# Splitting the output weights on TensorE while a delta-rule kernel inverts its first systems

## The reference, cut to what matters

```python
# attention by the delta rule, 2 x 8 heads, 768 tokens, head size 48
k_n = k / (np.linalg.norm(k, axis=-1, keepdims=True) + 1e-06)
for t in range(S):
    y[t] = q[t] @ state
    state = state + beta[t] * outer(k_n[t], v[t] - k_n[t] @ state)
# SoLU layer, 1536 rows, 384 -> 1024 -> 384
h = x @ w_in;  solu = h * softmax(h)
ln = (solu - mean) / sqrt(var + 1e-6) * g_ln
x = ln @ w_out
# router (x @ w_gate, best of 8) and one expert per row, 384 -> 1024 -> 384
```

## Time and profile before

| | us |
|---|---|
| median of 3 runs | 436.16 |
| lowest, highest | 435.88, 438.93 |
| the profiled execution, its own time | 435.01 |
| span of its records | 433.2 |
| PE busy, share of the span | 390.2, 90% |
| DVE busy | 311.4, 72% |
| ACT busy | 221.9, 51% |
| POOL busy | 66.6, 15% |

### The profile page before, as it was taken

The page is one execution under the profiler, slowest core; times in us unless marked ns, Lnnn a source line. Parts: engine busy times, 40 slices in busy tenths (PEclk is TensorE's granted clock), DMA queues, the critical chain, the costliest instruction groups (busy, mean ns, idle before and its releaser), DMA issues.

```text
span 433.2 us, 13384 instructions
## 1 busy us (share of the span) xinstructions
PE 390.2 (90%) x5617; PEld 371.1 (86%) x5618; DVE 311.4 (72%) x612; ACT 221.9 (51%) x393; POOL 66.6 (15%) x79
## 2 busy tenths in 40 slices
PE   3386789799999899999989998999999999999992
PEld 3386788779999888999877998999999999999991
DVE  6999699679957958883425887796596775647650
ACT  2437331647831226663124772577696594648650
POOL 3100200000020000010012000625144242210211
PEclk9999999999999969999999998999999999999997
DMA  7996001289100329101034941246738738080000
GB/s 152 328 227 176 5 2 36 50 160 314 70 34 10 74 70 209 34 21 40 5 77 123 395 175 38 56 145 225 285 76 305 249 129 315 26 309 21 25 5 26
DMA packets 27878, 54.37 MB, mean 125 GB/s; under 512 B 4468, under 2 KB 21424, under 8 KB 27344
## 3 DMA queue, kind: packets, MB, share of 16 engines
q1 hardware_dynamic: 23648, 48.04, 36.9%
q0 software_dynamic: 3136, 4.73, 3.5%
q10 hardware_dynamic: 1040, 0.79, 0.8%
HBM read 44.30 MB, written 9.44 MB: 124 GB/s over the span
## 4 chain that ended last, share of the span: by engine, by line
PE 74%; DVE 14%; issue 5%; SPq 2%; DMA 2%; ACT 1%; POOL 1%; POOLq 0%; DVEq 0%
PE PS L542 10%; PE PS L544 10%; PE PS L543 10%; PE PS L1509 8%; PE PS L1554 4%; PE PS L1564 3%; PE PS L1555 3%; PE PS L1438 3%; PE PS L1395 3%; PE PS L1424 2%; PE PS L1412 2%; PE PS L1521 2%; PE PS L1372 2%; SPq L269 2%; PE PS L1346 2%
## 5 line engine op out<-in xcount | busy, mean ns | idle before, releaser
L542 PE MATMUL PS<-xTh,w1h 128*128 128x224 f32 (+3 forms) x198 | 55.8, 282 | 0.6 <-DVE hTl L451 0.6
L543 PE MATMUL PS<-xTl,w1h 128*128 128x224 f32 (+3 forms) x198 | 55.5, 281 | 0.0
L544 PE MATMUL PS<-xTh,w1l 128*128 128x224 f32 (+3 forms) x198 | 55.5, 281 | 0.0
L1509 PE MATMUL PS<-w_in_h,mlpT 128*128 128x512 f32 x144 | 47.7, 404 | 0.9 <-DMA mlpT<-yT 0.7
L542 PE MATMUL PS<-w2h,hTh 128*128 128x384 f32 x136 | 46.2, 340 | 0.0
L544 PE MATMUL PS<-w2h,hTl 128*128 128x384 f32 x136 | 45.6, 335 | 0.0
L543 PE MATMUL PS<-w2l,hTh 128*128 128x384 f32 x136 | 45.5, 335 | 0.0
L451 DVE SCALAR_TENSOR_TENSOR hTl<-PS,hTh 128x384 fp32r<-128x384 f32 x64 | 35.5, 554 | 4.7 <-ACT hTh L349 4.7
L542 PEld LDWEIGHTS PS<-xTh,w1h 128*128 128x128 f32 x198 | 38.0, 192 | 1.0 <-DVE hTl L451 1.0
L477 POOL DMA_INDIRECT out<-yo,oiu x24 | 24.0, 999 | 92.6 <-ACT yo L360 84.7
L544 PEld LDWEIGHTS PS<-xTh,w1l 128*128 128x128 f32 x198 | 38.0, 192 | 0.0
(11 more groups left out here) (190 smaller groups left out, 908.6 us busy)
## 6 DMA issues: line engine op xcount, KB each, us to landing
w1r<-w SPq DMA_DIRECT2D x8, 1536.0 KB, 6.5
w2r<-w SPq DMA_DIRECT2D x8, 1536.0 KB, 10.8
KP<-kv SPq DMA_DIRECT2D x3, 1536.0 KB, 13.3
mlpT<-yT SPq DMA_DIRECT2D x12, 288.0 KB, 4.3
QT<-qt SPq DMA_DIRECT2D x6, 384.0 KB, 6.4
out<-zero SPq DMA_DIRECT2D x12, 192.0 KB, 3.9
x<-rowst SPq DMA_DIRECT2D x12, 192.0 KB, 1.9
XE<-w_out_t SPq DMA_DIRECT2D x1, 1536.0 KB, 6.4
```

The costliest lines, as they stand in the source:

```text
L542: pe.matmul(out_ap, lhs[0], rhs[0], start=first, stop=False)
L543: pe.matmul(out_ap, lhs[0], rhs[1], start=False, stop=False)
L544: return pe.matmul(out_ap, lhs[1], rhs[0], start=False, stop=final)
L1509: last = pe.matmul(PS[:, h_bank(n) + s, :], mlpT[:, n, x, c, :], w[:, c, o], start=(c == 0 and j == 0), stop=(c == KD - 1 and j == 2))
```

## The change

1. PE makes the low part of `w_out`: for each of 8 slices it multiplies the identity with the scaled `w_out` (f32, 384 columns) and the negated identity (`minus`) with `w_out_h` (fp32r), both into one PSUM bank, in four calls `w_out_low(0..3)` of two slices. ACT copies each call's result to `w_out_l`. ACT makes `w_out_h` in two halves. The subtraction at L1207 shrinks to the 64 columns of the router's part.
2. New orders. PE: `w_out_low(0)`, `w_out_low(1)`, `fold`, `w_out_low(2)`, `grams(1)`, `w_out_low(3)`, a wait for ACT's last copy, 8 products of zeros, `between(0)`, 4 products of zeros, `lower_block(0)`. `grams(1)` waits for ACT's part of `fold`. ACT: `w_out_high(0)`, `w_out_high(1)`, the copies of `w_out_low(0)` and `(1)`, `fold`, copy 2, `w_in_high` (moved up from `attention(0)`), copy 3, `odd_blocks(1)`, `between(0, 0)`, `lower_rows(0)`, `between(0, 1)`, `lower_block(0)`, `cross_blocks(1)`, `roots(1)`. DVE: after `place_rows(0)` a copy of block 1 that was ACT's, `scale_v(0)`, a wait for ACT's `lower_rows(0)`, a memset of block 3 that was POOL's, `lower_block(0)`, and only then `systems(1)` and `mask_first`.
3. The joining products go in halves of 16 units, so that the taking out of one half lies beside the products of the other; this holds for all groups.
4. The norms: ACT computes the square with the epsilon and the plain sum in two small instructions after the root (`Square` and `Identity` with a bias tile `tiny`), in place of two of DVE's.
5. `T1u` is stored as [block position, unit] in place of [unit, block position]: DVE's transposition writes in order, and PE reads its 32 columns 128 bytes apart.
6. The first DVE memset of PSUM is cut in halves, so that `grams(0)` waits for the first only; the copies of its odd blocks are cut in quarters, the first two taken half-way through the products.
7. SP issues `g_ln` and `w_out` first, then the keys of group 1, `w_gate`, `w_out_t`, `kv`, `w_in`.

```diff
+                sp.dma_start(gl[:], g_ln).then_inc(ld_wo, 16)
+                sp.dma_start(w_raw[:, :, 0:DM], w_out.rearrange("(k p) n -> p k n", p=P)).then_inc(ld_wo, 16)
+                load_kt(1)
+                sp.dma_start(wg[:], w_gate.rearrange("(c p) e -> p c e", p=P)).then_inc(ld_wt, 16)
                 sp.dma_start(w_out_t_sb, w_out_t.rearrange("(c p) f -> p c f", p=P)).then_inc(ld_wt, 16)
-                sp.dma_start(wg[:], w_gate.rearrange("(c p) e -> p c e", p=P)).then_inc(ld_wt, 16)
-                sp.dma_start(gl[:], g_ln).then_inc(ld_wt, 16)
-                sp.dma_start(w_raw[:, :, 0:DM], w_out.rearrange("(k p) n -> p k n", p=P)).then_inc(ld_wt, 16)
-                load_kt(1)
                 load_kv(0)
...
-                act.activation(nq[:], flat[:, 0:BL * BL:BL + 1], ACT.Sqrt).then_inc(root_done, 1)
+                act.activation(nq[:], flat[:, 0:BL * BL:BL + 1], ACT.Sqrt).then_inc(root_step, 1)
...
+                act.activation(nq2[:], nq[:], ACT.Square, bias=tiny[:]).then_inc(root_done, 1)
+                act.activation(nq1[:], nq[:], ACT.Identity, bias=tiny[:]).then_inc(root_done, 1)
...
 (ACT's list)
+                act.wait_ge(ld_wo, 32)
+                w_out_high(0)
+                w_out_high(1)
+                w_out_low(0)
+                w_out_low(1)
                 fold()
+                w_out_low(2)
+                w_in_high()
+                w_out_low(3)
                 odd_blocks(1)
+                between(0, 0)
                 lower_rows(0)
-                between(0)
+                between(0, 1)
+                lower_block(0)
+                cross_blocks(1)
                 roots(1)
-                cross_blocks(1)
-                lower_block(0)
...
 (DVE's list)
                 place_rows(0)
+                dve.wait_ge(td_ready, 1)
+                dve.tensor_copy(TT64[block(1), :, 1], TT64[block(1), :, 0]).then_inc(d_tb, 1)
                 scale_v(0)
+                dve.wait_ge(e_tb, 1)
+                dve.memset(TT64[block(3), :, 0], 0.0).then_inc(z_tt, 1)
+                lower_block(0)
+                systems(1)
                 mask_first()
-                systems(1)
-                lower_block(0)
                 dve.wait_ge(w_hi, 1)
-                dve.tensor_tensor(w_out_l[:], w_raw, w_out_h[:].bitcast(F32), ALU.subtract).then_inc(w_lo, 1)
+                dve.tensor_tensor(w_out_l[:, :, DM:RW], w_raw[:, :, DM:RW], w_out_h[:, :, DM:RW].bitcast(F32), ALU.subtract).then_inc(w_lo, 1)
...
 (PE)
+                def w_out_low(i):
+
+                    pe.wait_ge(w_main, i // 2 + 1)
+                    if i >= 2:
+                        pe.wait_ge(w_low_main, i - 1)
+                    for k in range(2 * i, 2 * i + 2):
+                        at = low_at(i)[:, k % 2]
+                        pe.matmul(at, ident[:], w_raw[:, k, 0:DM], start=True, stop=False)
+                        last = pe.matmul(at, minus, w_out_h[:, k, 0:DM], start=False, stop=True)
+                    last.then_inc(w_diff, 1)
...
+                w_out_low(0)
+                w_out_low(1)
                 fold()
+                w_out_low(2)
                 grams(1)
+                w_out_low(3)
+                pe.wait_ge(zero_ready, 1)
+                pe.wait_ge(w_low_main, 4)
+                idle_products(8)
                 between(0)
+                idle_products(4)
                 lower_block(0)
```

More of the change, by code:

```diff
@@ L720, in clear_t @@
                 def clear_t(g):
[L722 to L725, removed]
+                    if g == 0:
+                        pool.wait_ge(d_tb, 1)
+                    for c in range(1 if g == 0 else 2):
+                        if g:
+                            pool.wait_ge(e_tb, 2 * g + c)
+                        pool.memset(TT64[block(2 * c + 1), :, 0], 0.0).then_inc(z_tt, 1)
                 def strictly_lower(g):
@@ L749, in odd_blocks @@
                 def odd_blocks(g):
[L751 to L754, removed]
+                    if g == 0:
+                        b = block(1)
+                        for i in range(2):
+                            if i:
+                                act.wait_ge(kk, 4)
+                            else:
+                                act.wait_ge(k_half, 4)
+                            for par in range(2):
+                                o = bank_of_grams(2 * par + i)
+                                last = act.activation(o[b, :, 0:BL], o[b, :, BL:CH], ACT.Copy)
+                    else:
+                        act.wait_ge(kk, 4 * (g + 1))
+                        for c in range(2):
+                            b = block(2 * c + 1)
+                            last = act.activation(grams_at(g)[b, :, 0:BL], grams_at(g)[b, :, BL:CH], ACT.Copy)
                     last.then_inc(a_od, 1)
@@ L774, in lower_rows, with between @@
                     act.wait_ge(td_ready, g + 1)
-                    for c in range(2):
+                    for c in range(1 if g == 0 else 0, 2):
                         b = block(2 * c + 1)
[L777 to L783, removed]
+                        act.activation(TT64[b, :, 1], TT64[b, :, 0], ACT.Copy).then_inc(e_tb, 1)
+                def between(g, h):
+                    o = slice(NU // 2 * h, NU // 2 * (h + 1))
+                    act.wait_ge(m1, 4 * g + 2 * h + 2)
+                    act.activation(M1s[:, o], blocks_at[:, o], ACT.Copy, scale=-1.0).then_inc(e_m1, 1)
                 def lower_block(g):
-                    act.wait_ge(pp, 2 * (g + 1))
-                    act.activation(TT64[block(0), :, 1], blocks_at[block(0)], ACT.Copy).then_inc(e_tt, 1)
+                    for h in range(2):
+                        act.wait_ge(pp, 4 * g + 2 * h + 2)
+                        act.activation(joined_in(TT64[block(0)], h), blocks_of(block(0), h), ACT.Copy).then_inc(e_tt, 1)
                 def take_scores(g):
@@ L910, in mlp @@
                         lower_rows(g + 1)
-                        between(g + 1)
+                        between(g + 1, 0)
+                        between(g + 1, 1)
                     mlp_rows(g, 2)
@@ L1038, in lower_block @@
                 def lower_block(g):
[L1040 to L1041 removed]
+                    for h in range(2):
+                        dve.wait_ge(pp, 4 * g + 2 * h + 2)
+                        dve.tensor_copy(joined_in(TT64[block(2)], h), blocks_of(block(2), h)).then_inc(d_tt, 1)
                 def solution(g, n):
@@ L1175, in slots @@
                     dve.sem_inc(slots_ready, 1)
-                dve.memset(PS[:, :, :], 0.0).then_inc(ps_clear, 1)
+                for k in range(2):
+                    dve.memset(PS[:, 4 * k:4 * k + 4, :], 0.0).then_inc(ps_clear, 1)
                 dve.memset(St[:], 0.0).then_inc(s_clear, 1)
-                dve.wait_ge(const_ready, 5)
+                dve.wait_ge(const_ready, 6)
                 for par in range(2):
@@ L1309, in grams @@
                     if g == 1:
-                        pe.wait_ge(e_pt, 1)
+                        pe.wait_ge(wfolded, 1)
                     elif g:
@@ L1323, in grams @@
                                     last.then_inc(kk, 1)
+                                if g == 0 and i == HP // 2 - 1:
+                                    last.then_inc(k_half, 1)
                 def scores(g):
```

124 lines of the change are left out of this document (82 added, 42 removed).

## The result

The changed kernel takes 448.95 us (median of 4 runs, 448.69 to 450.48) against 436.02 for the kernel before beside it (4 runs, 431.08 to 438.93). The measured ratio is 1.034, with an interval of 1.025 to 1.043; the medians alone give 1.030. The profiled execution took 448.69, its span is 446.9 against 433.2, so the traces differ by 13.7 us. The kernel before, run 26 times beside some of the experiments, went from 431.5 to 444.3. A profile shows only where one execution spent its time.

The account below looks back on a forecast made before the run. The prediction took the kernel as TensorE-bound, DVE leading in the inversion and up to the first `solution`. Terms +1.15, +0.1 and +0.65 made +1.9 us on the median 436.16, so 438.0 us, range 431.5 to 443.

Parts of the forecast that it names:

- `T1u` read 128 bytes apart: ... I take 0: Joining products of all groups: PE's scattered operand costs 0, bounded by 0 and twice 2.14 us in three groups, +6.4.
- a rival with chance 0.1: Joining products: the strided operand costs what the line rule says, +2 us in each group, 443 us in all; chance 0.1.
- The 17 ns: Joining products: 2.14 / 128 = 17 ns for a product of 32 columns, taken as 1 ns a column, supporting 0 cost.
- The forecast's sum in group 0: Whole change: +1.15 up to the joining's end, +0.1 to the first `solution`, +0.65 behind it, +1.9 us.
- `fold` at 10.4 us: PE's 48 `fold` products at the lower clock, from about 26.3 to 36.7 us; 5.2 if the clock were up.
- PE's queue comes earlier: Rival: dense products raise the clock in `fold`, `between(0)` starts at 43.1 to 44, total 434.7 or 432 us; chance 0.25.
- `w_out_low` at 1.6 us a call: PE's low-part products in front of `between(0)`: 0.8 us a slice, two slices a call, from bounds of 0.72 to 1.1.
- my upper bound: PE's f32 product with 384 columns: at most three times an idle product of 128 columns, 3 x 0.25 = 0.75 us.
- From there to the end of the half copy: Group 0 joining, from `between(0)` at 46.3 to the end of `lower_block(0)`'s copies at 52.0: 5.7 us, before 11.4.
- Joining: I take the upper level: Group 0 joining: after dense calls and idle products PE runs at the upper clock, 2.14 us for 128 products.
- Halves at 0: Groups 1 and 2: joining in halves keeps the same products and ACT copy total, added small instructions lie beside PE: 0.
- A delay D comes out at the end as about D: First `solution` of group 0: PE leads almost without a hole from there, so a delay or gain passes through.

Follow-up runs that it names:

- run 26: No label but a count: the kernel before, unchanged, was run 26 times beside some of the experiments, from 431.5 to 444.3 us.
- e1: The changed kernel with `T1u` stored again so that PE reads its columns in order, nothing else differing: 440.08 us (433.17 to 445.29) beside 437.19 for the kernel before.
- e2: The kernel before with only `T1u` stored position by unit, columns 128 bytes apart: 441.75 us, 1.012 times the kernel before.
- e12: The kernel before with `T1u` in blocks of 4 units, so PE reads columns 16 bytes apart: 442.73 us, 1.021 times the kernel before.
- e6: The changed kernel with `T1u`'s columns in order and without the 8 and 4 products of zeros: 439.16 us, 1.011 times the kernel before.
- e5: The changed kernel with `T1u`'s columns in order and `mask_first` and `systems(1)` moved back into DVE's idle time: 438.45 us, 1.006 times the kernel before.
- e3: The kernel before with DVE's 3.4 us subtraction to `w_out_l` done twice: 444.78 us beside 437.19, ratio 1.017.
- e9: The kernel before with the subtraction done twice, plus 14 products of zeros in PE's idle time behind `solve(0, 3)`: 443.28 us beside 436.64, ratio 1.018.
- e8: The kernel before with parts 4 and 6, `fold` waiting only for its own weights, DVE order `systems(1)`, `mask_first`, subtraction, `lower_block(0)`: 434.18 us, ratio 0.998.

## Why the prediction was wrong, point by point

**The step that failed** is "`T1u` read 128 bytes apart: ... I take 0". It was a rival with chance 0.1, and even there its price was the direct one only, 443 in all against 448.95 measured. The direct part was 3.73 - 2.14 = 1.6 us in groups 1 and 2, inside the bounds of 0 to 2.14. What the sum had no term for is that the clock can fall right behind these products, which added 1.4 to 2 us in one of the two groups. Undone (e1), the two runs that count are back in the range of the kernel before; alone (e2, e12) the operand gives 1.012 and 1.021. The two readings by which I chose 0 were poor. The 17 ns are those of one record, and a product has two (33 ns); either says nothing of what a scattered operand adds. DVE's 1.2 ns for a scattered element were read at L970 from PSUM, and `T1u` lies in SBUF; they say nothing of PE's read. The Trainium skill (SBUF — State Buffer, Door 1: The DMA port swizzle) says that each access to a new line of 16 bytes pays a penalty. By that the operand had to cost, and it did; its allowance that f32 may be strided by 4 elements for free does not hold for this operand, as e12's 3.94 us show.

**The forecast's sum in group 0** was +1.9 at the first `solution` and behind it; it is +5.03 there. By its terms:

- `fold` at 10.4 us: it took 7.95, since the clock was up when it began (25.63, 0.65 for two records) and fell during it (0.81 from 28 to 29 us, 0.50 behind). This was the start of the rival "PE's queue comes earlier".
- `w_out_low` at 1.6 us a call: a call takes 3.2 us at the lower level (1.28 + 0.32 a slice), and the last one took 1.85 at the upper. The earlier trace rows are 4 products in 8 records, so my upper bound was half of what a product of zeros told. The two errors cancel: `between(0)` starts at 45.17, forecast 46.3.
- From there to the end of the half copy: 9.84 us, forecast 5.7. `between(0)` 3.73 instead of 2.14 (the operand), 1.79 of products of zeros that I had called hidden (the copies they were to fill end before them), `lower_block(0)` 3.60 instead of 2.14 (the clock fell at 49.1; in e1 it did not). "Joining: I take the upper level" held for the clock at the start, and not for the time.
- From there to the first `solution`: 6.92, forecast 6.15. The subtraction of 64 columns took 1.20, not 0.3. In the kernel after, e1 and e6, POOL's selection ran beside `mask_first` and this subtraction and took 3.23 to 3.24 us, and the subtraction 1.27 (1.20 of them in the chain); in e5, where they lay apart, 1.27 and 0.22. So the two cost each other time when they meet, and the sum had no term for it.
- The transposition to `T1u` took 1.94 us, not the 1.26 of L970, so `T1u` was ready at 38.2, not at 36 to 37; nothing waited for it.
- Halves at 0: the way through group 1 has no fall of the clock in any profile with halves, and one in each without; that is 4.07 us in the pair of before and after, in the favour of the change.
- Right: `T1u` ready is followed by a wait of PE of 7 us; DVE's 3.42 us go and 1.25 + 2.17 come (`systems(1)` and `mask_first` are in the chain; e5 takes them out and brings the first `solution` forward); the moved `w_in_high` holds nobody; PE idles before `gate` (2.15 us, forecast 3.5).

**"A delay D comes out at the end as about D"** failed too. 3.4 us cost 7.6 (e3) and 6.6 (e9) by the medians; the interval of e9 (5.4 to 10.6) excludes 3.4, that of e3 just touches it. And 3.7 us of gain behind `gate` in e8 left 2.1 by the medians, 0.9 by the ratio, and that not told from none. In every profiled kernel but the kernel before the clock fell somewhere between 60 and 97 us, and the step from the products behind `gate` to the first SoLU products took 22.7 to 25.0 us in all of them, against 21.34 in the profile of the kernel before, the shortest of all. Why the clock falls there stays open: filling one hole (e9) took away one fall of two. It may also be that the profile of the kernel before was a lucky one in this stage; its own runs spread by more than this.

**So the 13.7 us** divide as follows. Up to the first products behind `gate` 5.03. With ordered columns (e1) the joining is 3.8 us shorter (1.6 in `between(0)`, 0.7 in the products of zeros, 1.5 in `lower_block(0)`), but e1 began it 1.26 later and reached this point only 1.12 earlier; 3.91 of the 5.03 stay in it, with the orders of PE's queue and DVE's list. From there to the transpositions of group 0: 4.95, with falls of the clock at 69 and 86 us whose cause is open. In the two steps with the joining of groups 1 and 2: 4.47, the operand, with one fall of the clock; this part is shown. In group 1: -4.07, which goes with the halves. From the transpositions of group 2 on: 3.32. Part of this shows ahead of the experts, where the clock read 0.62 and 0.70 from 280 to 290 us, against 0.77 and 0.89 from 265 to 275 in the profile of before; why, I didn't trace, and the other profiles differ there as well.

## What to carry to other kernels

Keep TensorE's streamed f32 operand in order, even if another engine must write it scattered: the writer lost next to nothing by it, and at the upper level of the clock the reader paid 1.7 times, and in some groups the clock of what followed. Before moving work from one engine's list to another's, ask what the stage waits for: here the inversion's result already waited for PE, so nothing saved ahead of it could count, and what was freed on DVE was filled by what the new order put there. And price a shift of a stage with a change that only shifts (an instruction done twice), for a delay of 3.4 us cost about twice that by the medians.

## What the runs showed of the hardware beyond that

- 64 f32 products 32x32x32 (128 records) with the moving operand's columns 4, 16 and 128 bytes apart: 2.14, 3.94 and 3.73 us at the upper level of the clock (e1 and before, e12, after and e2). At the lower level: 3.88 us busy with 4 bytes (before), 4.07 with 128 (e2).
- The clock can fall behind such slow products with PE 100% busy: in the kernel after at 49 and 202 us, in e2 at 126. Of the eight joinings of groups 1 and 2 with scattered columns four show it, of the twenty with ordered ones none.
- An f32 product of 128x128 with 384 columns: 1.28 us at 1.2 GHz and 0.65 at 2.4, in two records; the fp32r product of the same size 0.32 and 0.18.
- DVE's transposition 128x1024 in f32, SBUF to SBUF, took 1.99 to 2.21 us with a scattered read and a scattered write (L1014 before), 1.94 to 2.06 with the read alone scattered (L1081 after) and 1.91 to 2.02 with the write alone (L1020 before); reading PSUM (L970) it took 1.25.
- POOL's selection 128x1024 took 1.27 us, and 3.23 where DVE instructions with two inputs from SBUF ran beside it; DVE's subtraction of 64 columns took 0.22 us, and 1.27 there (e5 against after, e1 and e6).
